# Alternating the products with the two weight matrices of a feed-forward layer, one by one, on TensorE

## What is computed

```python
h = x @ w_in
g = np.where(h >= 1, h, np.where(h <= -1, 0.0, (h + 1) ** 2 / 4))   # layer 0
x = g @ w_out
h = x @ w_in2
g = h - np.tanh(h)                                                   # layer 1
out = g @ w_out2
```

## Time and profile before

| | us |
|---|---|
| median of 3 runs | 797.55 |
| lowest and highest of them | 797.17 and 797.69 |
| the profiled execution, its own time | 796.39 |
| the span of its trace | 794.4 |
| of it, feed-forward from the first steady hidden product (263.7) to the last output product (789) | 525 |
| TensorE busy in the span | 765.7 |

### The profile page before, as it was taken

One profiled execution on the slowest core, in us unless ns is written; L12 is line 12 of the kernel. 1 busy time (PEld: TensorE's weight loads), 2 busy tenths in 40 slices (PEclk: granted clock), 3 DMA queues, 4 the chain that ended last, 5 costly groups with the idle time before them and its releaser, 6 DMA issues.

```text
span 794.4 us, 11750 instructions
## 1 busy us (share of the span) xinstructions
PE 765.7 (96%) x3712; PEld 637.0 (80%) x3712; DVE 422.4 (53%) x757; ACT 355.0 (45%) x701; POOL 326.3 (41%) x267
## 2 busy tenths in 40 slices
PE   4999999999999999999999999999999999999997
PEld 2788888888888788878887888778888888888885
DVE  2999999999996665343334455541213222222222
ACT  2888889889885333333334323331212212222121
POOL 4789889899899993000000267760000000000000
PEclk8999999999999999999999999999999999999999
DMA  5533423433132332000000022210001000010001
GB/s 193 179 103 112 152 78 116 145 104 104 61 98 80 133 110 78 0 1 1 0 1 0 26 86 99 98 61 1 1 0 42 11 0 0 0 53 0 0 0 53
DMA packets 17864, 47.25 MB, mean 59 GB/s; under 512 B 2288, under 2 KB 4464, under 8 KB 17840
## 3 DMA queue, kind: packets, MB, share of 16 engines
q1 hardware_dynamic: 17840, 46.94, 18.4%
HBM read 38.87 MB, written 3.15 MB: 53 GB/s over the span
## 4 chain that ended last, share of the span: by engine, by line
PE 80%; POOL 5%; issue 5%; DVE 4%; ACT 3%; DMA 2%; SPq 1%; DVEq 0%; POOLq 0%; ACTq 0%
PE ps L489 33%; PE ps L564 30%; PE ps L466 5%; PE ps L480 5%; PE ps L452 2%; PE ps L455 2%; PE ps L423 2%; POOL probs L346 2%; POOL k_b L331 1%; ACT probs L610 1%; DMA k_raw<-kk 1%; DVE g_raw L805 1%; ACT g_hi L692 1%; DVE row_den L735 1%; POOL q_b L303 1%
## 5 line engine op out<-in xcount | busy, mean ns | idle before, releaser
L489 PE MATMUL ps<-x_hi,w 128*128 (+1 forms) x768 | 255.0, 396 | 0.0
L813 DVE TENSOR_TENSOR g_lo<-g_raw,g_hi 128x512 fp32r<-128x512 f32 x96 | 72.4, 754 | 268.5 <-ACT g_hi L692 268.5
L692 ACT ACTIVATE g_hi<-g_raw 128x512 fp32r<-128x512 f32 x96 | 60.8, 633 | 294.9 <-PE ps L564 266.3
L489 PEld LDWEIGHTS ps<-x_hi,w 128*128 128x128 f32 x768 | 144.4, 188 | 33.9
L489 PE MATMUL ps<-x_lo,w 128*128 (+1 forms) x384 | 152.1, 396 | 0.0
L564 PE MATMUL ps<-g_hi,w 128*128 128x512 f32 x384 | 125.6, 391 | 3.1 <-DVE g_lo L813 3.1
L564 PE MATMUL ps<-w,g_hi 128*128 128x512 f32 x384 | 118.6, 390 | 0.0
L303 POOL TENSOR_SCALAR w<-stage 128x1024 fp32r<-128x1024 f32 x32 | 38.1, 1191 | 165.4 <-PE ps L564 163.5
L743 DVE TENSOR_TENSOR p_lo<-ps,p_hi 128x384 fp32r<-128x384 f32 x192 | 97.8, 551 | 9.6 <-ACT p_hi L620 7.7
L346 POOL TENSOR_SCALAR probs<-probs,row_inv 128x768 f32<-128x768 f32 x96 | 86.9, 909 | 23.5 <-DVE row_inv L737 23.5
L620 ACT ACTIVATE p_hi<-ps 128x384 fp32r<-128x384 f32 x192 | 84.7, 489 | 24.3 <-PE ps L466 22.7
(11 more groups left out here) (48 smaller groups left out, 900.8 us busy)
## 6 DMA issues: line engine op xcount, KB each, us to landing
stage<-weights SPq DMA_DIRECT2D x32, 512.0 KB, 3.3
qk_raw<-qk SPq DMA_DIRECT2D x16, 384.0 KB, 3.5
q_raw<-qq SPq DMA_DIRECT2D x16, 384.0 KB, 3.2
k_raw<-kk SPq DMA_DIRECT2D x16, 384.0 KB, 3.8
q_a<-q_b SPq DMA_DIRECT2D x16, 192.0 KB
v_raw<-v SPq DMA_DIRECT2D x16, 192.0 KB, 2.4
out<-stage SPq DMA_DIRECT2D x12, 256.0 KB, 2.3
q_b<-bits SPq DMA_DIRECT2D x16, 54.0 KB
```

What stands on the lines that cost most here:

```text
L489: last = nc.tensor.matmul(ps[:, f % H_BANKS, :], w[:, f, wp, k * P:(k + 1) * P], xs[:, :, k, bass.ds(t * TOK, TOK)], start=(k == 0 and wp ...
L692: nc.scalar.activation(g_hi[:, slot, :], g_raw[:, slot, :], ACT.Copy).then_inc(g_hi_ready, 1)
L813: nc.vector.tensor_tensor(g_lo[:, slot, :], g_raw[:, slot, :], g_hi[:, slot, :].bitcast(F32), ALU.subtract).then_inc(g_split, 1)
```

## The change

The loop over the 16 steps calls no `hidden` and `project` any more where both are due. It makes the waits of both at the head of the step, and then twenty-four products in turn: one hidden product, one output product, and so on. The semaphore increments stay on the last product of either kind (h_ready, y_step). The first four `hidden` of a tile, the early ones, and the last four steps of a tile are as before. The operands, the banks and the order within each kind are the same.

```diff
--- before.py
+++ after.py
@@ -483,13 +483,17 @@
                 if r == HT - 1:
                     last.then_inc(pv_ready, 1)
 
+            def hidden_product(t, f, k, i):
+
+                wp, xs = ((0, x_hi), (0, x_lo), (1, x_hi))[i]
+                return nc.tensor.matmul(ps[:, f % H_BANKS, :], w[:, f, wp, k * P:(k + 1) * P],
+                                        xs[:, :, k, bass.ds(t * TOK, TOK)],
+                                        start=(k == 0 and i == 0), stop=(k == KC - 1 and i == 2))
+
             def hidden_part(t, f, k):
 
-                for wp, xs in ((0, x_hi), (0, x_lo), (1, x_hi)):
-                    last = nc.tensor.matmul(ps[:, f % H_BANKS, :], w[:, f, wp, k * P:(k + 1) * P],
-                                            xs[:, :, k, bass.ds(t * TOK, TOK)],
-                                            start=(k == 0 and wp == 0 and xs is x_hi),
-                                            stop=(k == KC - 1 and wp == 1))
+                for i in range(3):
+                    last = hidden_product(t, f, k, i)
                 return last
 
             def early_hidden(i):
@@ -540,7 +544,7 @@
             for m in range(4):
                 pe.sem_inc(out_copied[m], 1)
 
-            def project(layer, t, f):
+            def project_waits(layer, t, f):
 
                 step = FC * (TT * layer + t) + f
                 pe.wait_ge(g_split, step + 1)
@@ -550,22 +554,22 @@
                     pe.wait_ge(y_free, 1 + KC * TT)
                     for m in range(4):
                         pe.wait_ge(out_copied[m], 1 + t)
-                for m in range(4):
-                    cols = slice(m * P, (m + 1) * P)
-                    wide = slice(KC * P, CH)
-                    narrow = slice((KC + m) * P, (KC + m + 1) * P)
-                    if layer == 0:
-                        products = [(w[:, f, 0, narrow], g_hi[:, f % 2, :]), (w[:, f, 0, narrow], g_lo[:, f % 2, :]),
-                                    (w[:, f, 1, narrow], g_hi[:, f % 2, :])]
-                    else:
-                        products = [(g_hi[:, f % 2, cols], w[:, f, 0, wide]), (g_hi[:, f % 2, cols], w[:, f, 1, wide]),
-                                    (g_lo[:, f % 2, cols], w[:, f, 0, wide])]
-                    for i, (a, b) in enumerate(products):
-                        last = nc.tensor.matmul(ps[:, 4 + m, :], a, b, start=(f == 0 and i == 0),
-                                                stop=(f == FC - 1 and i == 2))
-                last.then_inc(y_step, 1)
-
-            def hidden(layer, t, f):
+
+            def project_product(layer, f, m, i):
+
+                cols = slice(m * P, (m + 1) * P)
+                wide = slice(KC * P, CH)
+                narrow = slice((KC + m) * P, (KC + m + 1) * P)
+                if layer == 0:
+                    a, b = [(w[:, f, 0, narrow], g_hi[:, f % 2, :]), (w[:, f, 0, narrow], g_lo[:, f % 2, :]),
+                            (w[:, f, 1, narrow], g_hi[:, f % 2, :])][i]
+                else:
+                    a, b = [(g_hi[:, f % 2, cols], w[:, f, 0, wide]), (g_hi[:, f % 2, cols], w[:, f, 1, wide]),
+                            (g_lo[:, f % 2, cols], w[:, f, 0, wide])][i]
+                return nc.tensor.matmul(ps[:, 4 + m, :], a, b, start=(f == 0 and i == 0),
+                                        stop=(f == FC - 1 and i == 2))
+
+            def hidden_waits(layer, t, f):
 
                 step = FC * (TT * layer + t) + f
                 pe.wait_ge(w_ready, FC * layer + f + 1)
@@ -575,6 +579,10 @@
                     pe.wait_ge(g_ready, step - H_BANKS + 1)
                     if f == 0:
                         pe.wait_ge(y_free, 1 + KC * (t + 1))
+
+            def hidden(layer, t, f):
+
+                hidden_waits(layer, t, f)
                 for k in range(KC):
                     last = hidden_part(t, f, k)
                 last.then_inc(h_ready, 1)
@@ -582,9 +590,18 @@
             def token_tile(layer, t):
 
                 for f in range(FC):
-                    if f + HEAD < FC:
-                        hidden(layer, t, f + HEAD)
-                    project(layer, t, f)
+                    ahead = f + HEAD < FC
+                    if ahead:
+                        hidden_waits(layer, t, f + HEAD)
+                    project_waits(layer, t, f)
+                    for m in range(4):
+                        for i in range(3):
+                            if ahead:
+                                h_last = hidden_product(t, f + HEAD, m, i)
+                            y_last = project_product(layer, f, m, i)
+                    if ahead:
+                        h_last.then_inc(h_ready, 1)
+                    y_last.then_inc(y_step, 1)
 
 
             pe.wait_ge(x_last_ready, 1)
```

## The result

The changed kernel takes 809.64 us (median of 5 executions, 807.53 to 809.95), the kernel before 797.49 in the same comparison: 12.2 us more, a ratio of 1.0147 with a 95% interval of 1.0134 to 1.0161. The forecast was 803.2 with a range of 799.2 to 808.2, so the result lies above the range. The sign and both places were right, both terms were too small. The profiled execution took 807.53 us, with a span of 805.6.

A forecast was written before the change was run, and what follows sets the result against it. TensorE's matmul pace was taken as the bound, busy 765.7 of 794.4 us. Moved wait +2.81 and alternation +2.9 gave +5.7 us, taking the median from 797.55 to 803.2 us, range 799.2 to 808.2.

The forecast's parts named there:

- Part 1: First tile's first step: the g_split wait moves ahead of twelve hidden products and loses their cover, +2.81 us; elsewhere covered.
- the clock's fall: Rival: the first step's 3.67 us idle time drops TensorE to half clock, +4.6 us on the forecast, 807.8; chance 0.12.
- a dense TensorE ahead of the gap: Argument against a clock drop at the first step: TensorE was dense before the new gap, unlike before the old 6.1 us one.
- The start time of 267.37: First tile's first step: output products start then, set by the gate's chain; with the change all twenty-four products start then.
- Part 2: Alternation in 6 tiles x 12 steps x 12 = 864 pairs of hidden and output products costs +2.9 us.
- I take the middle, 465 ns: Price of an alternating pair, between 461.0 and 469 ns; three products behind a switch share its surcharge.
- the named upper end of 469: Alternating steps: every change of kind pays what one pays now, 469 ns a pair, +6.3 us.
- Alternation free: Rival: in alternating steps each kind keeps its pace, leaving the moved wait and -0.6 us, 799.8; chance 0.17.
- the kinds help each other: Rival: output products let slow hidden fetches catch up, a pair 453.6 ns, -7.0 us, total 793.4; chance 0.10.
- the two stretches: Hidden products' moving operand comes in two stretches; a lagging fetch might make them 7.4 ns slower than output products.
- Dearer than single switches: Rival: alternating steps cost more than single switches show, 480 ns a pair, 816.2 us; chance 0.08.
- The wait does not come forward: Rival: the queue lets hidden products past the g_split wait, leaving only the alternation's cost, 800.4 us; chance 0.03.

The follow-up runs named there:

- e1: Kernel before, with only the very first step's g_split wait moved ahead of its hidden products, runs of twelve kept: 803.13 us, ratio 1.0069.
- e5: The change with the first two steps of the first tile put back in runs of twelve: 804.3 us, ratio 1.0089 to the kernel before.
- e17: The change as it is, all steps alternating, with w placed 58880 bytes behind x: 793.16 us, ratio 0.9941 to the kernel before.
- e3: The change with TensorE's token-tile loops unrolled, so that every operand has a fixed address: 810.19 us.
- e4: The change with the first tile's first step in runs of twelve, other steps in turns of three hidden and three output products: 800.21 us, ratio 1.0037.
- e10: Kernel before, with the 48 hidden products at the head of the five later tiles each writing another bank than the one before: 806.26 us.
- e9: Kernel before, with the PSUM bank groups of hidden and output products exchanged in layer 1: 802.98 us.
- e16: The alternating kernel of e5 (first two steps in runs of twelve) with w 58880 bytes behind x: 788.58 us, ratio 0.9891 to the kernel before.
- e6: Kernel before, with output products ordered so that each writes another PSUM bank than the one before, runs of twelve kept: 797.47 us, ratio 1.0001.
- e7: Kernel before, with the hidden products' moving operand read as one stretch of 512 columns instead of two of 256: 797.52 us, ratio 0.9998.
- e8: The alternating kernel of e5 with the moving operand read as one stretch of 512 columns: 805.07 us, ratio 1.0100 to the kernel before.
- e14: The alternating kernel of e5 with x moved 32 bytes further, w 58496 bytes behind x: 796.07 us, ratio 0.9988 to the kernel before.
- e15: Kernel before, in its old order, with an unused 416-byte buffer placing w 58880 bytes behind x: 788.61 us, ratio 0.9885.
- e12: Kernel before, with x moved 32 bytes further, w 58496 bytes behind x: 796.26 us, ratio 0.9991.
- e13: Kernel before, with x in place and w, g moved 32 bytes further, w 58496 bytes behind x: 796.08 us, ratio 0.9986.
- e18: Kernel before, in its old order, with w 58624 bytes behind x: 788.42 us, ratio 0.9880.
- e2: The change with only the first step of the first tile put back in runs of twelve: 806.54 us, ratio 1.0116 to the kernel before.

## Why the prediction was wrong

**The bound.** Right: TensorE's pace decides, 3712 matmuls with 10.2 us more busy time. The two places that the prediction named are the two places of the loss (e1 and e5 add up to the change).

**Part 1, +2.81 us, measured 5.7 (e1) and 4.6 (e17).** The mechanism held: one wait at the first step, the cover of twelve products gone, none in the steady steps and none at the tiles' heads. The 2.81 us themselves fit. The term was mis-sized by the sentence that put the clock's fall apart, as a rival with a chance of 0.12. The wait of 3.9 to 4.6 us brought a stretch at 1.2 GHz in each of the four profiled executions with it (change, e1, e3, e17). It is part of the term, and not a rival to it. Its price was named as 4.6 us; measured by the long distances behind the restart it was 1.5 us in the profile of the change, 2.9 in e1 and e3, 2.1 in e17. The argument that a dense TensorE ahead of the gap speaks against it was worth nothing. The start time of 267.37 was taken as fixed, which it is not: the products started at 267.80, 268.04 and 269.65 (change, e1, e17). Only 0.3 to 0.9 us of that is a longer wait than in the forecast, 3.67 us; in e1 and e17 TensorE also reached the step 0.4 and 1.4 us later.

The Trainium skill, "TensorE: Matmul & The Clock Gate", section "HAM oscillation — how this bites in real kernels", was on the right side here: it says that idle time between bursts of matmuls puts the array back to half clock. The traces agree for every idle time of 2.5 us and more in the feed-forward part (2.46 us in e4, 2.52 in e10, 3.6 in e9, 3.9 to 4.6 in the four above); behind the shorter ones, up to 1.7 us in e16 and 1.8 in e10, the clock stayed at 1.00.

**Part 2, +2.9 us, measured 6.7 for 70 steps (e5); 72 steps of 0.100 us make 7.2.** The step that failed is "I take the middle, 465 ns". The steady value is 470 ns, just over the named upper end of 469. The middle rested on sharing the surcharge among three products behind a switch. In a strict alternation nobody recovers, and the stream settles into a rhythm of its own, 235 ns per matmul, or more rarely 232 or 233; the share of a product behind a switch told nothing of that. The point before it, that the order of banks is free, was right (e6).

**The rivals.** "Alternation free" and "the kinds help each other" were wrong for this kernel, and their common assumption about the two stretches fell in e7 and e8. With x at another distance the first comes true, e14 and e16 alternate for nothing. The second does not: the hidden products reach 226.7 ns there without an output product between them (e15). "Dearer than single switches" was the right direction with the wrong size (480 ns, measured 470); the clock stayed at 1.00 throughout the steady steps, and changing the bank cost nothing (e6). "The wait does not come forward" fell in the order and in the trace.

**The range.** It ended at 808.2 because it took the upper end of part 2 and the fall of the clock one at a time. Added, 2.8 + 6.3 + 4.6 us, they give 811.

The prediction noticed that hidden products took 7.4 ns more and gave it to the two stretches without a test. That unexplained difference was the key to the surcharge and to 9 us of the kernel before. It also weighed a rule of the Trainium skill, "TensorE: Matmul & The Clock Gate", section "Back-to-back issue gap". That section gives N/2.4 + 2.5 ns, 216 ns here, as the gap of an isolated matmul, and for a stream of weight loads and matmuls a distance set by both, about 131 ns. That the neighbour does not matter is the prediction's reading of the formula. No run here reaches either figure: the shortest distance is 226.7 ns, and only at the distances of e15, e16 and e18 have both kinds the same. The Trainium skill, on the same page, section "Step-by-step: what each phase is for", says of loading weights beside a running matmul that it "doesn't steal SBUF read bandwidth". Within a run of hidden products only x (moving) and w (weights) are read at a distance that is no multiple of 256, and the pace of the run hangs on that distance (e12, e13, e15, e18); so the two reads do not run free of each other at 58464 bytes. By what mechanism the runs do not show. In the alternation x also lies at that distance from g and, in layer 1, from w as a moving operand; no run changed one of these distances without the others, so which pair makes the surcharge stays open.

Open too is what chooses between the rhythms; of the alternating profiles at 58464 bytes, the change's first tile had 232 ns per matmul, e8's first tile 233, and all other tiles 235.

## What to carry to other kernels

- When two kinds of matmul with the same columns differ in pace by a few ns, find out why before predicting what a mixture does; try the operands' distance in a partition first, with an unused buffer, which costs one line. Here a multiple of 256 bytes was worth 9 us of 797.
- A wait moved ahead of work loses the work as its cover, and an idle TensorE can pay again in clock: here all seven feed-forward waits of 2.5 us and more did, with 1.5 to 2.9 us each. Count both in one term, and look at the next step too, where the wait can reappear (e2, e4).
- A surcharge seen at single switches was not divided here when every product was a switch (470 ns a pair, against 469 by the undivided surcharge): take the upper end.

## What the runs showed of the hardware that was not expected

- The pace of a 512-column float32r matmul at the full clock was 234.2, 233, 227 ns, depending on the distance between x and w: 58464, 58496, and 58624 or 58880 bytes. Moving x or moving w gave the same (e12, e13).
- At 58464 bytes alternating with matmuls of the other kind slowed those too, to 235 ns for all; at 58496 it cost nothing (5.520 us per step against 5.527).
- A strict alternation at 58464 bytes ran in one of several steady rhythms: eight matmuls in 1.88 us in nearly all tiles, six in 1.39 in the change's first tile, and steps of 5.600 us in e8's.
- TensorE gaps of 2.46 us (e4) and 2.52 us (e10) were followed by matmuls 0.43 us apart, beginning 0.8 and 1.0 us after the restart; gaps of up to 1.8 us were not (e10).
